# Gates by tanh in each step, one slot matrix for all experts, weight loads spread over the steps, and spare TensorE products

## The reference

```python
# 1: a gated recurrence; B=4, H=8, S=768, D=40
for t in range(S):
    m_new = maximum(f_gate[t] + m, i_gate[t]); f = exp(f_gate[t] + m - m_new); i = exp(i_gate[t] - m_new)
    C = f * C + i * outer(v[t], k[t]);  n = f * n + i * k[t]
    y[t] = sigmoid(o_gate[t]) * (C @ q[t]) / maximum(abs(n @ q[t]), 1)
x = y as (3072 tokens, 320)
# 2: eight experts with 4 slots each (32 slots)
logits = x @ phi                                  # (3072, 32)
slot_input = softmax(logits, tokens).T @ x        # (32, 320)
slot_out[e] = relu(slot_input[e] @ w1[e]) @ w2[e] # w1 (320, 1024), w2 (1024, 320)
x = softmax(logits, slots) @ slot_out             # (3072, 320)
# 3: feed-forward
out = square(relu(x @ w_in)) @ w_out              # w_in (320, 2048), w_out (2048, 320)
```

## Time and profile before

| what | value |
|---|---|
| runs (3) | 417.29, 419.45 (median), 423.09 us |
| profiled execution, its time | 420.38 us |
| its span | 418.7 us |
| mean granted clock of PE | 0.947 |
| busy share | PE 89%, PE weight loads 74%, DVE 59%, ACT 52%, POOL 20% |
| moved | 54.85 MB |

### The profile page before, as it was taken

How to read it: one execution, slowest core, us unless ns; L and a number is a source line. 1 busy time by engine, 2 the same in 40 slices (tenths; PEclk the granted TensorE clock), 3 DMA queues, 4 the chain that set the end, 5 groups by cost and what they waited for, 6 DMA issues and landing times.

```text
span 418.7 us, 9229 instructions
## 1 busy us (share of the span) xinstructions
PE 371.7 (89%) x3404; PEld 311.7 (74%) x3404; DVE 245.1 (59%) x569; ACT 216.2 (52%) x381; POOL 84.4 (20%) x102
## 2 busy tenths in 40 slices
PE   0179999879989989689958999999999999999996
PEld 0167777658767767332427999999999999999996
DVE  8426879822795797540164556556556556556553
ACT  5844455333345554303045666656666666566653
POOL 6036656324473663000050000000000000000000
PEclk9999999985699999759995999999999999999999
DMA  7838769997569750999930001001001001001001
GB/s 236 311 81 223 220 198 315 332 238 184 159 218 271 201 157 9 357 363 378 292 111 2 2 1 64 0 2 63 0 0 63 0 0 63 0 0 56 10 0 64
DMA packets 31379, 54.85 MB, mean 131 GB/s; under 512 B 2544, under 2 KB 22704, under 8 KB 31024
## 3 DMA queue, kind: packets, MB, share of 16 engines
q1 hardware_dynamic: 31344, 54.38, 42.0%
HBM read 49.86 MB, written 4.42 MB: 130 GB/s over the span
## 4 chain that ended last, share of the span: by engine, by line
PE 73%; DVE 11%; DMA 9%; SPq 3%; ACT 2%; issue 2%; POOL 0%; DVEq 0%
PE heads_banks L1055 7%; PE heads_banks L1056 7%; PE high_banks L1056 7%; PE high_banks L1055 7%; PE high_banks L1057 7%; PE heads_banks L1057 7%; PE low_banks L1043 5%; PE low_banks L773 5%; PE heads_banks L794 5%; DMA qk_in<-in_qk 4%; PE low_banks L967 3%; DMA wo_raw<-in_w_out 3%; PE high_banks L809 2%; PE heads_banks L787 2%; PE low_banks L825 2%; PE low_banks L762 2%
## 5 line engine op out<-in xcount | busy, mean ns | idle before, releaser
L720 ACT ACTIVATE relu_h<-low_banks 128x512 f32<-128x512 f32 x96 | 57.5, 599 | 67.9 <-PE low_banks L1043 67.6
L1354 DVE CAST sq_hi<-sq_h 128x512 fp32r<-128x512 f32 x96 | 41.0, 427 | 74.6 <-ACT sq_h L725 74.0
L1356 DVE TENSOR_TENSOR sq_lo<-sq_h,sq_hi 128x512 fp32r<-128x512 f32 x96 | 66.5, 693 | 3.3
L725 ACT ACTIVATE sq_h<-relu_h 128x512 f32<-128x512 f32 x96 | 60.7, 632 | 3.0
L1055 PE MATMUL heads_banks<-wo_hi,sq_hi 128*128 128x320 f32 x192 | 60.0, 313 | 1.8 <-DVE sq_lo L1356 1.8
L1056 PE MATMUL heads_banks<-wo_lo,sq_hi 128*128 128x320 f32 x192 | 59.9, 312 | 0.0
L1055 PE MATMUL high_banks<-wo_hi,sq_hi 128*128 128x320 f32 x192 | 59.8, 311 | 0.0
L1056 PE MATMUL high_banks<-wo_lo,sq_hi 128*128 128x320 f32 x192 | 59.8, 311 | 0.0
L1057 PE MATMUL high_banks<-wo_hi,sq_lo 128*128 128x320 f32 x192 | 59.8, 311 | 0.0
L1057 PE MATMUL heads_banks<-wo_hi,sq_lo 128*128 128x320 f32 x192 | 59.6, 310 | 0.0
L1096 DVE TENSOR_TENSOR att_w<-low_banks,att_w 128x512 f32<-128x512 f32 x48 | 30.9, 686 | 34.4 <-PE low_banks L773 21.1
(11 more groups left out here) (163 smaller groups left out, 527.0 us busy)
## 6 DMA issues: line engine op xcount, KB each, us to landing
w_sb<-in_w SPq DMA_DIRECT2D x8, 1280.0 KB, 14.3
w_a<-in_w SPq DMA_DIRECT2D x8, 1024.0 KB, 10.1
qk_in<-in_qk SPq DMA_DIRECT2D x48, 160.0 KB
kv_in<-in_kv SPq DMA_DIRECT2D x24, 320.0 KB, 6.7
fade_b<-fade_scratch SPq DMA_DIRECT2D x40, 80.0 KB
out<-out_sb SPq DMA_DIRECT2D x5, 640.0 KB, 3.2
wo_raw<-in_w_out SPq DMA_DIRECT2D x4, 640.0 KB, 12.7
w_b<-in_w SPq DMA_DIRECT2D x8, 256.0 KB, 11.4
```

The source lines that it names most:

```text
L720: act.activation(relu_h[:, slot], bank[slot][:, :], ACT.Relu).then_inc(relu_done, 1)
L725: act.activation(sq_h[:, slot], relu_h[:, slot], ACT.Square).then_inc(sq_done, 1)
L1354: dve.tensor_copy(sq_hi[:, slot], sq_h[:, slot]).then_inc(hi_done, 1)
L1356: dve.tensor_tensor(sq_lo[:, slot], sq_h[:, slot], sq_hi[:, slot].bitcast(F32), ALU.subtract).then_inc(lo_done, 1)
```

## The change

**Gates.** `o_gate` is loaded per step (160 KB, two steps ahead, ring of three). `half_tanh` on ACT, after `copy_heads` and ahead of `copy_xT`, takes the tanh of half of it, in two instructions of 128x160. `denominators` makes 2 x (heads times sigmoid) as (tanh + 1) x heads in one instruction, and doubles the denominators.

**Loads.** From the step 1 on, each of 16 steps issues one 512 KB piece of `w1`, and each second one 256 KB more; expert 0's `w2` follows in the step 17, expert 1's when batch 2's slots are summed (`slots_summed` 3). The other six come behind the last steps. `w_in` now waits for `hidden` 4, as `w_out` does.

**Start.** Exp table first; fade's exp ahead of keyw's; the scratch stores and some loads moved up; `log_i` on POOL waits for `log_f` instead of `m_run`.

**Spare products.** `stay_awake(count)` does fp32 products of the identity with `consts` (256 columns) into a bank nobody reads then.

**Rebuilt way.** `slot_acc` isn't scaled or padded: the scale goes into `fold_scaled`. `slotsT` holds all 32 slots once, every expert is computed for all of them, and `fold_own` picks each expert's own four when the outputs are turned. `expert_first(n)` covers all eight experts; its last, 64-row products run for both groups g, in the array's two row halves. DVE takes half of the relus. `outsT` is copied on ACT. Each `w1_b` holds four experts below four others. `turn_x` and `logit` use 64 rows or columns in the third piece. DVE's split of part 1 and ACT's high parts of 2 and 3 (`raise_w_out`) move into the first token block, behind f = 1, and f = 1 and 3.

```diff
-            for c in loads(1):
-                load_w1(W1_EARLY[2 * c:2 * c + 2])
...
+            for n in range(STEPS):
+                b, c = n // NC, n % NC
...
+                    load_qk(*far)
+                    load_kv(*far)
+                if n + 2 < STEPS:
+                    load_o(*after(*after(b, c)))
+                if 0 <= n - W1_FIRST_STEP < 2 * E:
+                    load_w1_main(*W1_PARTS[n - W1_FIRST_STEP])
+                    if (n - W1_FIRST_STEP) % 2 == 1:
+                        load_w1_rest((n - W1_FIRST_STEP) // 2)
+                if n == W1_FIRST_STEP + 2 * E:
+                    load_w2(0)
+
+            sp.wait_ge(slots_summed, B - 1)
+            load_w2(1)
...
+            for e in range(W2_AHEAD, 6):
+                load_w2(e)
             sp.wait_ge(heads, STEPS)
...
+            for e in range(6, E):
+                load_w2(e)
-            sp.wait_ge(hidden, 2)
+            sp.wait_ge(hidden, 4)
             sp.dma_start(win_sb[:, 0:2], ...
...
-            pool.wait_ge(gate_vec, G_M)
+            pool.wait_ge(gate_vec, G_LOGF)
...
+            def half_tanh(b, c):
+                n, s = step(b, c), c % 3
+                act.wait_ge(o_loaded[s], 16 * (n // 3 + 1))
+                at_least(act, x_ready, n - 1)
+                for odd in range(2):
+                    own = slice(2 * odd, 2 * (odd + 1))
+                    ins = act.activation(gates[:, c % 2, own], paired(o_in[:, s], odd), ACT.Tanh, scale=0.5)
+                ins.then_inc(gate_ready, 1)
...
+                    if isinstance(tb, int) and tb == 0 and f in (1, 3):
+                        raise_w_out((f + 3) // 2)
...
+            def stay_awake(count, spare=heads_bank):
+                for _ in range(count):
+                    pe.matmul(spare[:, 0:2 * P], ident, consts[:, :], start=True, stop=True)
...
+            pe.wait_ge(gate_vec, G_CUM)
+            stay_awake(11)
             decay(0, 0)
...
+            stay_awake(2)
...
+                if (b, c) == (0, 0):
+                    stay_awake(3)
                 if cur:
                     attend(b, c)
...
-            pe_step(B, 0, 0, nxt=False, cur=False)
+            stay_awake(5)
+            turn_x(B - 1, NC - 1, 1)
+            stay_awake(2)
+            pe.wait_ge(decay_exp, step_exps(B - 1, NC - 1))
+            logit(B - 1, NC - 1)
+            stay_awake(1)
             turn_logits(B - 1)
+            stay_awake(1)
...
             turn_disp(B - 1)
-            sum_slots(B - 1, 1)
+            stay_awake(1)
+            sum_slots(B - 1, 1, range(TRI))
...
+            sum_slots(B - 1, 1, range(TRI, NC))
+            stay_awake(1)
+            pe.wait_ge(scale_folded, 1)
+            pe.wait_ge(slots_added, 2 * B)
             for k in range(KC):
-                mm = pe.matmul(turned_bank[:, ...], slot_acc[:, P * k:P * (k + 1)], fold[:, 0:QUAD], ...
+                mm = pe.matmul(turned_bank[...], slot_acc[:, P * k:min(P * (k + 1), DM)], fold_scaled[:, :], ...
...
+            def expert_first(n):
+                for g in range(2):
+                    for k in range(2):
+                        for q in range(4):
+                            pe.matmul(bank[2 * g + n][QUAD * q:QUAD * (q + 1), :], slotsT[:, k], w1_a[:, 4 * g + q, k, 512 * n:512 * (n + 1)],
+                                      start=k == 0, stop=False)
+                for q in range(4):
+                    for g in range(2):
+                        rows = slice(DP * g, DP * g + DM_LAST)
+                        mm = pe.matmul(bank[2 * g + n][QUAD * q:QUAD * (q + 1), :], slotsT[rows, 2], w1_b[rows, q, 512 * n:512 * (n + 1)],
+                                       start=False, stop=True)
+                mm.then_inc(hidden, 2)
...
+            expert_first(0)
+            turn_comb(B - 1, 0)
+            expert_first(1)
+            turn_comb(B - 1, 1)
+            turn_hidden(0, 0)
+            turn_hidden(1, 0)
             pe.wait_ge(w2_loaded[0], 64)
             expert_second(0, 0)
+            turn_hidden(0, 1)
...
             expert_second(1, 1)
+            stay_awake(1, bank[3])
             turn_outs(1)
+            stay_awake(2, bank[3])
...
+            stay_awake(4, bank[0])
             pe.wait_ge(spread_ready, 2)
...
+            stay_awake(2, bank[0])
             pe.wait_ge(sw_ready[0], 1)
...
+                    if first and f == 0:
+                        stay_awake(5, bank[3])
...
+                dve.scalar_tensor_tensor(out=x_gated..., in0=gates[:, c % 2]..., scalar=1.0, in1=turned_ps..., op0=ALU.add, op1=ALU.mult)
...
+            add_sums(B - 1)
+            dve.wait_ge(slots_added, 2 * B - 1)
+            scale_thirds()
+            dve.tensor_scalar(fold_scaled[:, :], fold[0:TS, 0:QUAD], slot_scale[:, 0:1], None, ALU.mult)
+            add_slots(B - 1)
+            dve.wait_ge(slots_turned, 1)
+            dve.tensor_copy(slotsT[:, :, :], turned_bank[...])
...
+                    if isinstance(tb, int) and tb == 0 and f == 1:
+                        split_w_out(1)
```

More of the change, by code:

```diff
@@ L30 @@
 FADE_RING = 3
+W2_AHEAD = 2
 WO_PART = 4
@@ L440, in _ @@
             sp.wait_ge(rows_direct, 128)
-            def loads(b, last=False):
-                for c in range(NC):
-                    if c == 1 and not last:
-                        load_src(b + 1)
-                    if not (last and c + 3 >= NC):
-                        far = (b, c + 3) if c + 3 < NC else (b + 1, c + 3 - NC)
-                        if step(*far) >= ROW_RING:
-                            load_rows(*far)
-                        if far[1] > 0 and far != (0, 3):
-                            load_fades(*far)
-                        load_qk(*far)
-                        load_kv(*far)
-                    yield c
@@ L457, in _ @@
[L457 to L470 removed]
+            for n in range(STEPS):
+                b, c = n // NC, n % NC
+                if c == 1 and b + 1 < B:
+                    load_src(b + 1)
+                if n + 3 < STEPS:
+                    far = after(*after(*after(b, c)))
+                    if step(*far) >= ROW_RING:
+                        load_rows(*far)
+                    if far[1] > 0 and far != (0, 3):
+                        load_fades(*far)
+                    load_qk(*far)
[8 more added lines that the diff above has]
+                    load_w2(0)
@@ L646, in _ @@
             copy_v(0, 0)
-            for b in range(1, B):
-                sigmoid(b)
-            act.preload_act_table(ACT.Exp)
+            act.activation(fade[:, :], cum[:, :], ACT.Exp).then_inc(gate_act, 1)
             act.wait_ge(gate_vec, G_KEYW)
@@ L652, in _ @@
             decays(0, 0)
-            act.activation(fade[:, :], cum[:, :], ACT.Exp).then_inc(gate_act, 1)
             def act_step(b, c, half, nxt=True, cur=True, prev=True, rb=None):
@@ L1076, in pe_block @@
                     out_tile(tb, f)
-            for i in range(2):
-                pe.wait_ge(sw_ready[i], 2)
             pe_block(0, first=True)
@@ L1281, in _ @@
             dve.tensor_reduce(thirds[:, :], ident.rearrange("p (q s) -> p q s", q=4), AX.X, ALU.add)
+            dve.wait_ge(fold_cleared, 1)
+            for e in range(E):
+                rows, own_slots = slice(QUAD * (e % 4), QUAD * (e % 4 + 1)), slice(SLOTS_PER_E * e, SLOTS_PER_E * (e + 1))
+                ins = dve.tensor_copy(fold_own[rows, e // 4, own_slots], fold[rows, own_slots])
+            ins.then_inc(fold_owned, 1)
             dve.wait_ge(keyw_turned, 1)
```

254 lines of the change are left out of this document (108 added, 146 removed).

## The result

| what | before | after |
|---|---|---|
| median (runs) | 418.80 us (4) | 429.37 us (4) |
| lowest to highest | 417.29 to 423.09 | 425.91 to 430.81 |
| span of the profiled execution | 418.7 | 426.4 |
| granted clock, mean | 0.947 | 0.944 |

The ratio is 1.0223, with a 95% interval of 1.0122 to 1.0325: slower beyond its noise, though by more than 2% or by less is not settled. Forecast had been 400 us, in a range of 388 to 410.

The account below looks back on a forecast made before the run. Bound by PE at low clock, PE waiting for `w1`, and the way to the feed-forward. 420.4 - 4.2 - 4.4 - 11.25 + 1.0 - 6.9 + 6.2 = 400.9, forecast 400 us, range 388 to 410.

Parts of the forecast that it names:

- The start: Up to the first attend: `row_y` lands sooner without `o_gate` ahead of it; gain 4.2 us, bounds 2 to 5.5.
- Clock in batch 0: First attend to batch 1's decay: steps at full clock if spare products keep PE at 2.4 GHz; gain 4.4 us.
- `w1` spread: Steps carrying `w1`: stall and low clock after it go, gain 11.25 us, against 1.0 us charged for the loads.
- transfers bound the steps: Rival, 16 steps: at 253 GB/s 1.64 MB take 6.5 us per step, 11 us more, 412 us; chance 0.12.
- Gates by tanh: Gates in each step: two tanh on ACT, hidden behind `turn_x`; 0 us, bounds 0 and 0.3 us on 24 steps.
- table-load rival: Steps on ACT: tanh and exp not in one table, two loads per step, 438 us; chance 0.03.
- Way to the feed-forward: End of the steps to the first relu: gain 2.9 + 3.6 + 0.4 = 6.9 us; bounds 4 and 10.
- First token block: From the first relu: DVE waits for POOL's splits, PE falls to half clock; tile 4 comes 6.2 us later.
- Two collisions: First token block: DVE waits for two POOL instructions, PE waits 6.1 us after tile 1; 400 us, chance 0.50.

Follow-up runs that it names:

- apart: Changed kernel with DVE's split of `w_out` part 1 ahead of `sw_cols` again and ACT's high parts behind tiles 2 and 6 of the first block: 425.33 us.
- no_spare: Changed kernel without any of the spare products: 434.85 us.
- w1_late: Changed kernel with all of `w1` and expert 0's `w2` loaded behind the last step's loads: 431.51 us.
- no_o: Changed kernel with `o_gate` loaded only for the first three steps, later gates reading those again: 415.01 us.
- alt: Changed kernel with only the order of the 256 KB `w1` pieces altered, so that neighbours lie in different partition halves: 429.35 us, 1.0276 times before.
- pairs_timed: Same kernel as `pairs`, timed in rounds against the kernel before: 420.36 us (4 runs), ratio 1.0024.
- best2: Changed kernel with `w1` in 20 paired 512 KB pieces, steps 1 to 20, both early experts' `w2` behind the loop, edits of `apart`: 399.65 us, 0.9561 times before.
- spread_apart: Changed kernel with 24 `w1` pieces over steps 1 to 22, 256 KB ones alternating, early `w2` behind the loop, edits of `apart`: 413.55 us, 0.9869 times before.
- w1_act: Changed kernel with the same pieces of `w1` at the same steps, issued by ACT on its own queue: 426.14 us.
- pairs: Changed kernel with the last 64 rows of `w1` of two experts as one 512 KB transfer to 128 partitions, four for eight: 420.5 us.

## Why the prediction was wrong

**The start held.** `row_y` took 2.04 us (2 said), the first decay came at 17.8 (18.2 said), the first attend at 22.6 (21.7 said). Attend follows the decay by 4.8 us where 3.5 was said, and the spare products between them hold most of it: three take 2.59 us there, at a granted clock of 0.62 from 20 to 22 us; in `apart`, whose start is the same, they take 1.56, and attend comes at 21.6. `log_i` on POOL took 3.05 us, from 7.57 on, in place of the 2.30 in the earlier trace rows.

**Clock in batch 0 held** but for 1.4 us: the first step still has a stretch at half clock (0.50 from 22 to 23 us), and the next two take 4.7 us each. `no_spare` is 4.0 us slower there, near the 4.4 said.

**"`w1` spread ... It just fits, with the loads two to three steps ahead; I charge 1.0 us" is the step that failed.** The gain that it set against this, 11.25 us for steps at their own pace, is right: `w1_late` shows 87.0 us for 16 steps where the sum had 87.7. The charge was wrong, and by the runs it is 20 us in place of 1.0 in these steps, and 7 more in the last batch:

- The rate of 335 GB/s is that of a stretch full of `w1`'s 1 MB pieces, at a share over 1. From 85 us on, behind the 64-row pieces (issued from 78.16 us on), the kernel before moved less, at a share of about 0.9:

```profile
85.00:90.00 5.00, 2.49 (x27) 1.97 (x26) 2.66 (x9) 1.47 (x3) 1.28 (x3) 1.00 0.92 223
90.00:95.00 5.00, 4.52 (x45) 3.38 (x47) 0.00 (x0) 1.08 (x2) 0.00 (x0) 0.67 0.86 195
```

  The mixture of a step moves 263 GB/s at a full share (234 / 0.89). At that, 1.64 MB take 6.2 us, and a step has 5.0 to 5.7. The second row had about the right price: 197 GB/s at 0.78, so 253.
- 8.5 to 10.6 of the 20 us go with `w1`'s last 64 rows (107.6 to 99.1, 108.7 to 98.1). The prediction counted these, 128 KB per step on average, by their bytes, and they take twice as long as such bytes to 128 partitions.
- 6.8 us are the gates, now 160 KB in every step that the transfers fill (`no_o`).

These overlap. What they do to PE is read from step 1 to 17 of each kernel, where PE does the same products (1223 or 1224 records). Windows after and of `w1_late`:

```profile
27.40:135.04 107.64, 92.90 (x1223) 69.02 (x1220) 61.95 (x185) 51.42 (x128) 46.57 (x59) 0.89 0.89 237
27.26:114.22 86.96, 82.32 (x1223) 62.80 (x1220) 68.25 (x185) 51.38 (x128) 48.15 (x60) 1.00 0.65 188
```

| kernel | us | PE busy | PE idle | mean granted clock |
|---|---|---|---|---|
| `w1_late` | 87.0 | 82.3 | 4.6 | 1.00 |
| after | 107.6 | 92.9 | 14.7 | 0.89 |
| `alt` | 108.7 | 98.6 | 10.1 | 0.83 |
| `apart` | 109.8 | 96.2 | 13.6 | 0.86 |
| `no_o` | 100.9 | 90.0 | 10.9 | 0.93 |
| `pairs_timed` | 98.1 | 90.7 | 7.4 | 0.91 |
| `best2` | 92.8 | 85.9 | 6.9 | 0.96 |

Longer busy time for the same products is the low clock, the rest is waiting. Of the 20.7 us after, 10.6 are clock and 10.1 waits; of `alt`'s 21.7, 16.3 are clock. So half or more of what the late loads cost is the low clock behind them, which the prediction's price, bytes by a rate, does not hold at all.

**Expert 0's `w2` in step 17 stood in the sum at no price.** The last batch went from 33.2 (`w1_late`) to 40.3 us, 7 more than said. Windows of it, after:

```profile
150.00:155.00 5.00, 2.89 (x41) 2.11 (x39) 3.79 (x14) 2.08 (x7) 1.75 (x3) 0.86 0.75 214
155.00:160.00 5.00, 5.00 (x44) 3.94 (x37) 1.90 (x6) 1.78 (x5) 3.05 (x4) 0.50 0.90 261
160.00:165.00 5.00, 5.00 (x49) 3.78 (x49) 4.40 (x10) 1.93 (x4) 3.06 (x5) 0.50 0.45 124
```

SP issued the 1280 KB at 140.25, ahead of the rows for step 21; the chain has those rows at 145.15 with 8.27 us. PE is busy for 2.89 of 5 us, and then runs at 0.50 for ten more while the transfers thin out (share 0.45): one stall, and its price paid in clock. The six executions with this piece in step 17 and all else as after in the last batch take 39.7 to 42.0 us; `best2` and `spread_apart`, without it there, 33.6 and 35.2, though the last pieces of `w1` are moved in their last batch. But `no_o` has 34.4 and `w1_act` 35.3, with the piece. It was not moved alone, so that it is the cause is argued, and stays open: what is shown is that 6.1 of the 7.1 us are low clock behind this stall (in the last batch PE is busy for 37.1 us, and for 31.0 in `w1_late`, with the same 458 products), and that less in SP's queue (`no_o`, `w1_act`) takes most of them away as well.

**The rival "transfers bound the steps" was the true one, and too cheap.** Its 104 us for 16 steps is close to 107.6, in part by luck: it has no term for the low clock, which is half of the loss. It then took 5 us off for the lead of a step, of which nothing was seen, and left out the last batch. Without the 5 and with the 7.4 it would have said 424. Its chance of 0.12 was set by "335 GB/s in the same mixture", but the mixture was not the same: of the eight 64-row pieces only two had been issued by the end of that window.

**Gates by tanh: right**, 0 us. The Trainium skill (ScalarE: Activation LUTs, Table sets: the hidden batching unit) lists tanh with exp, and the trace agrees: no table load stands in the steps after, the only one of the kernel is at 0.81 us. The table-load rival falls.

**Way to the feed-forward: right**, 6.9 us said and measured, and its parts within 0.3. Timeline of PE after: start us, us, instructions.

```profile
190.36 3.64 PE L992 MATMUL low_banks<-w_a,slotsT 128*32 128x512 f32 x32 [0.36 <-DVE slotsT L1349]
193.93 1.09 PE L997 MATMUL low_banks<-w_b,slotsT 64*32 64x512 f32 x16
...
195.43 3.64 PE L992 MATMUL low_banks<-w_a,slotsT 128*32 128x512 f32 x32
199.00 1.09 PE L997 MATMUL low_banks<-w_b,slotsT 64*32 64x512 f32 x16
```

From the end of the steps to the first expert product 15.0 us against 18.0 (2.9 said); from there to the product with `w_in` 25.2 against 28.5 (3.6 said); from there to the relu 6.9 against 7.5 (0.4 said). The 64-row parts of both groups take 1.09 us together, where one took 1.06: the two row halves of the array do work at the same time.

**First token block: right in mechanism, near in size.** Two collisions, as the timelines above show: a wait of 5.5 us (6.1 said), and 4.8 us lost of the 6.2 said. The Trainium skill (SBUF — State Buffer, SBUF: two separate sides) has an exclusive lock: whichever of the two engines starts first holds it for its whole instruction, and the other is blocked. The trace agrees both ways, for POOL's instructions are stretched too, 3.49 and 3.88 us in place of 2.90, and each began while one of DVE's ran (`L1371` until 226.70, `L1373` until 230.87). The prediction had only DVE wait. `apart` takes both collisions away.

## What to carry to other kernels

Price a load by the rate that its own kind reaches, not by the best window: ask how many partitions it goes to, and read a mixed stretch at its own share. Before loads are spread into a loop, compare bytes per turn over that rate with the turn's time; when they come out level, the loop is bound by transfers, each stall costs clock on top, and a lead of two or three turns does not absorb a deficit that recurs each turn. A tensor's ragged last rows are better laid out to full height, and what is not needed in the loop better issued behind it, up to the point where what follows it waits.

## What had not been expected of the hardware

- Pieces of 256 KB to 64 partitions at 194 to 227 GB/s, against 407 to 409 for pieces of 512 KB or 1 MB to 128.
- Pieces of the two heights mixed, two full and one half, move 262 GB/s, though by their rates apart they would make 338 (10.5 MB in 31 us). Why the mixture is worse than its parts was not settled. Within the steps, laying neighbouring half-height pieces on different sides changed nothing (`alt`).
- The same 24 steps differ by some 5 us from run to run when the transfers are full (152.7 and 157.5 us, after and `apart`); two runs of `pairs` have 144.5 and 144.1.
- The granted clock reads 1.00 at the start of the execution while the products take nearly twice as long (1.98 us for 16 in place of 1.09, `no_spare`).
- When DVE and POOL meet, both grow: together POOL's two and DVE's two took from 226.02 to 233.9 us, 7.9 us, against 2 x 2.90 + 1.49 + 0.43 = 7.7 by themselves, so they take turns and lose nothing more.
